# Slot logits in pairs of tiles, and the products with d in one group, in a fused attention and soft-MoE kernel

## What is computed

```python
# attention, 8 batches, 8 heads, 576 tokens, head dim 64; keys and values are pooled by 8 to 72
k_p = k.reshape(B, H, 72, 8, D).mean(axis=3); v_p = ...same...
attn = softmax(q @ k_p.T / sqrt(D))                 # 576 x 72 for each head
x = concat_heads(attn @ v_p)                        # 4608 x 512
# soft MoE, 32 slots
logits = x @ phi                                    # 4608 x 32
d = softmax(logits over the tokens)                 # one column for each slot
slot_in = d.T @ x                                   # 32 x 512
slot_out = relu(slot_in @ w1[e]) @ w2[e]            # 8 experts, 4 slots each
c = softmax(logits over the slots);  x = c @ slot_out
# SoLU layer
h = x @ w_in;  u = h * softmax(h);  out = layernorm(u) * g_ln @ w_out
```

## Time and profile before

| | us |
|---|---|
| median of 3 executions | 486.39 (486.37 to 488.03) |
| the profiled execution | 485.29 |
| its span in the trace | 483.4 |
| PE busy in the span | 442.7 |
| ACT busy | 251.1 |
| DVE busy | 318.9 |
| POOL busy | 271.1 |

### The profile page before, as it was taken

The page is one execution under the profiler, slowest core; times in us unless marked ns, Lnnn a source line. Parts: engine busy times, 40 slices in busy tenths (PEclk is TensorE's granted clock), DMA queues, the critical chain, the costliest instruction groups (busy, mean ns, idle before and its releaser), DMA issues.

```text
span 483.4 us, 10639 instructions
## 1 busy us (share of the span) xinstructions
PE 442.7 (92%) x3845; PEld 357.2 (74%) x3845; DVE 318.9 (66%) x518; ACT 251.1 (52%) x553; POOL 271.1 (56%) x359
## 2 busy tenths in 40 slices
PE   1879999999999997778886999999999999999996
PEld 0867888888888874456655888887878888888885
DVE  7666776868768772735408898767677777777411
ACT  2364758676686752110226765556556665666310
POOL 0397687777888230053812434657576666666540
PEclk9998999999999997898998999999999999999999
DMA  8969897798989447899800016666666666666652
GB/s 264 292 149 293 297 311 213 287 268 299 319 217 322 171 159 259 308 358 397 315 1 0 23 45 133 135 126 134 128 131 135 132 135 135 133 134 132 135 121 48
DMA packets 125296, 91.75 MB, mean 190 GB/s; under 512 B 104776, under 2 KB 104784, under 8 KB 123216
## 3 DMA queue, kind: packets, MB, share of 16 engines
q1 hardware_dynamic: 125264, 91.32, 68.2%
HBM read 66.13 MB, written 9.44 MB: 156 GB/s over the span
## 4 chain that ended last, share of the span: by engine, by line
PE 70%; SPq 11%; DVE 7%; issue 3%; DMA 3%; ACT 3%; POOL 2%; DVEq 0%
SPq L423 10%; PE banks L1373 9%; PE banks L1375 9%; PE banks L1374 9%; PE banks L1065 8%; PE banks L1117 5%; PE banks L1053 4%; PE banks L1133 3%; PE banks L1285 3%; PE banks L1169 3%; PE banks L1350 2%; PE banks L1097 2%; PE banks L1265 2%; PE banks L1141 2%; PE banks L1073 1%
## 5 line engine op out<-in xcount | busy, mean ns | idle before, releaser
L1373 PE MATMUL banks<-wo_hi,uh 128*128 128x512 f32 x288 | 112.5, 391 | 0.0
L1374 PE MATMUL banks<-wo_lo,uh 128*128 128x512 f32 x288 | 112.1, 389 | 0.0
L1375 PE MATMUL banks<-wo_hi,ul 128*128 128x512 f32 x288 | 112.0, 389 | 0.0
L537 POOL TENSOR_TENSOR ul<-u_col,uh 128x1024 fp32r<-128x1024 f32 x30 | 72.1, 2405 | 30.5 <-ACT uh L566 30.4
L457 POOL TENSOR_TENSOR attn<-attn,srec 128x576 f32<-128x576 f32 (+1 forms) x40 | 45.9, 1148 | 59.3 <-DVE srec L802 59.3
L734 ACT ACTIVATE sq<-u,usum 128x1024 f32<-128x1024 f32 x36 | 41.5, 1153 | 41.6 <-DVE u L986 41.5
L1375 PEld LDWEIGHTS banks<-wo_hi,ul 128*128 128x128 f32 x288 | 54.0, 188 | 11.3
L1374 PEld LDWEIGHTS banks<-wo_lo,uh 128*128 128x128 f32 x288 | 54.1, 188 | 11.1
L1373 PEld LDWEIGHTS banks<-wo_hi,uh 128*128 128x128 f32 x288 | 54.1, 188 | 11.1
L976 DVE TENSOR_REDUCE nmax<-banks 128x1 f32<-128x1024 f32 x36 | 43.6, 1220 | 20.0 <-PE banks L1350 20.0
L1065 PE MATMUL banks<-kblk,qT 128*128 128x144 f32 (+1 forms) x320 | 49.9, 302 | 4.8 <-issue 2.4
(11 more groups left out here) (159 smaller groups left out, 753.7 us busy)
## 6 DMA issues: line engine op xcount, KB each, us to landing
wslot<-in_moe_w SPq DMA_DIRECT2D x15, 2048.0 KB, 9.9
u_col<-u_blk SPq DMA_DIRECT2D x240, 64.0 KB, 2.1
qb<-in_q SPq DMA_DIRECT2D x32, 256.0 KB, 6.8
out<-osb SPq DMA_DIRECT2D x32, 256.0 KB, 2.6
kraw<-in_k SPq DMA_DIRECT2D x8, 640.0 KB, 8.9
vraw<-in_v SPq DMA_DIRECT2D x8, 640.0 KB, 5.8
kraw<-in_k SPq DMA_DIRECT2D x8, 512.0 KB, 7.9
vraw<-in_v SPq DMA_DIRECT2D x8, 512.0 KB, 3.9
```

What stands on the lines that cost most here:

```text
L537: pool.tensor_tensor(ul[par][:, :, :].rearrange("p c (q t) -> p (c q) t", q=4), v, uh[par][:, :, :].bitcast(F32).rearrange("p c (q t) -> p ...
L1373: pe.matmul(ps[4 + par], uh[par][:, c, :], wo_hi[:, c, :], start=(c == 0), stop=False)
L1374: pe.matmul(ps[4 + par], uh[par][:, c, :], wo_lo[:, c, :], start=False, stop=False)
L1375: last = pe.matmul(ps[4 + par], ul[par][:, c, :], wo_hi[:, c, :], start=False, stop=(c == FC - 1))
```

## The change

`GROUPS` puts the tiles of a batch into (0,1), (2,3) and (4). The transposed attention `aT` and the copy `lt` become single buffers with room for two tiles. `lt_t`, `lt_evac`, `l_t` and `logit_evac` run once for a group, in steps 2, 4 and 5 instead of all five; for a pair the five matmuls of `lt_t` have 256 columns, `lt_evac` copies 256 columns, and `l_t` is two matmuls. In steps 1 and 3, where `lt_t` stood ahead of `aT_t`, `aT_t` itself now waits for the copy of the tile before. `dat_t` runs for all five tiles at once in step 3, ahead of the scores of that step; its three places of before are gone. `kT_t` moves ahead of `lmax_t` in step 1. Loads that waited for the old counts wait for the new ones. ACT's stream keeps its order and loses `lt_evac` in steps 1 and 3.

```diff
+GROUPS = [(0, 1), (2, 3), (4,)]
-        lt = [bump(f"lt{i}", [P, P]) for i in range(2)]
+        lt = bump("lt", [P, 2 * P])
-        aT = [bump(f"aT{i}", [P, NB, P]) for i in range(2)]
+        aT = bump("aT", [P, NB, 2, P])
...
@@ ACT
-            def lt_evac(tile):
-                n = ROWS[tile[2]]
-                act.wait_ge(sem("lt_ps"), num(tile) + 1)
-                copy(lt[bit(tile)][:, 0:n], b_lt[:, 0:n]).then_inc(sem("lt_sb"), 1)
+            def lt_evac(b, par, g):
+                act.wait_ge(sem("lt_ps"), groups(b, g) + 1)
+                cols = slice(0, 2 * P) if g < 2 else slice(bit((b, par, 4)) * P, bit((b, par, 4)) * P + ROWS[4])
+                copy(lt[:, cols], b_lt[:, cols]).then_inc(sem("lt_sb"), 1)
...
             def step(b, par, t, first, last):
...
-                if not (first and t == 0):
-                    lt_evac(ahead(b, par, t - 1))
+                if t in (2, 4, 5):
+                    lt_evac(b, par, group(t - 1))
...
@@ DVE
-                    sub_max(ahead(b, par, t + 2), None if t != 3 or first else dat_count(b - 1, 0))
+                    sub_max(ahead(b, par, t + 2), None if t != 3 or first else b)
-                if not (first and t == 0):
-                    logit_evac(ahead(b, par, t - 1))
+                if t in (2, 4, 5):
+                    logit_evac(b, group(t - 1))
...
@@ PE
             def aT_t(tile):
...
+                if t in (1, 3):
+                    pe.wait_ge(sem("aT_sb"), g * 2)
                 pe.wait_ge(sem("attn_ready"), g + 1)
...
+            def lt_t(b, par, g, early=False):
+                tiles = [(b, par, t) for t in GROUPS[g]]
+                pe.wait_ge(sem("aT_sb"), num(tiles[-1]) * 2 + 2)
+                if g == 0:
+                    pe.wait_ge(sem("vphi_sb"), b + 1)
+                if not early:
+                    pe.wait_ge(sem("l_sb"), groups(b, g))
                 for k, m in enumerate(BLOCKS):
+                    q = k % 4
+                    if len(tiles) == 2:
+                        o, i = b_lt[32 * q:32 * (q + 1), 0:2 * P], aT[0:m, k, :, :].rearrange("p a n -> p (a n)")
+                    else:
+                        c, n = bit(tiles[0]), ROWS[tiles[0][2]]
+                        o, i = b_lt[32 * q:32 * (q + 1), c * P:c * P + n], aT[0:m, k, c, 0:n]
+                    last = pe.matmul(o, vphi[par][0:m, k, :], i, start=(k < 4), stop=(k + 4 >= NB), tile_position=(0, 32 * q))
                 last.then_inc(sem("lt_ps"), 1)
...
             def step(b, par, t, first, last):
...
                     qT_t(ahead(b, par, t + 3))
-                if t == 4 and not first:
-                    dat_t(b - 1, 1 - par, (4,))
+                if t == 3 and not first:
+                    dat_t(b - 1, 1 - par)
                 if not (last and t + 2 >= TILES):
                     scores(ahead(b, par, t + 2))
+                if t == (2 if first else 1) and not last:
+                    kT_t(b + 1)
                 if not first:
                     if t == 1:
                         lmax_t(b - 1, 1 - par)
                     if t == 2:
                         mb_t(b - 1, 1 - par)
-                    if t == 3:
-                        dat_t(b - 1, 1 - par, (0, 1))
                     if t == 5:
                         slot_t(b - 1, 1 - par)
-                if t == (2 if first else 1) and not last:
-                    kT_t(b + 1)
-                if not (first and t == 0):
-                    lt_t(before, first and t == 1)
+                if t in (2, 4, 5):
+                    lt_t(b, par, group(t - 1), first and t == 2)
                 aT_t(tile)
-                if not (first and t == 0):
-                    l_t(before)
+                if t in (2, 4, 5):
+                    l_t(b, par, group(t - 1))
                 if t == 2 and not first:
                     v72_t(b)
-                if not first:
-                    if t == 3:
-                        dat_t(b - 1, 1 - par, (2, 3))
-                    if t == 4:
-                        datT_t(b - 1)
+                if t == 4 and not first:
+                    datT_t(b - 1)
```

More of the change, by code:

```diff
@@ L281, in c4_batches, with group, groups @@
             return range(2 * (e - 4), 2 * (e - 3)) if e >= 4 else range(0)
-        def dat_count(b, t):
-            return b * 3 + (1 + t // 2)
+        def group(t):
+            return t // 2
+        def groups(b, g):
+            return b * len(GROUPS) + g
         def made(i, k):
@@ L673, in _ @@
             datT_evac(B - 2)
-            lt_evac((B - 1, 1, 4))
+            lt_evac(B - 1, 1, 2)
             d_exp(B - 1)
@@ L1120, in aT_t, with l_t @@
                         last.then_inc(sem("aT_ps"), 1)
[L1122 to L1127, removed]
+            def lt_t(b, par, g, early=False):
+                tiles = [(b, par, t) for t in GROUPS[g]]
+                pe.wait_ge(sem("aT_sb"), num(tiles[-1]) * 2 + 2)
+                if g == 0:
                     pe.wait_ge(sem("vphi_sb"), b + 1)
                 if not early:
-                    pe.wait_ge(sem("l_sb"), g)
+                    pe.wait_ge(sem("l_sb"), groups(b, g))
                 for k, m in enumerate(BLOCKS):
-                    g = k % 4
-                    last = pe.matmul(b_lt[32 * g:32 * (g + 1), 0:n], vphi[par][0:m, k, :], aT[bit(tile)][0:m, k, 0:n],
-                                     start=(k < 4), stop=(k + 4 >= NB), tile_position=(0, 32 * g))
-                last.then_inc(sem("lt_ps"), 1)
[L1137 to L1141, removed]
+                    q = k % 4
[5 more added lines that the diff above has]
+                    last = pe.matmul(o, vphi[par][0:m, k, :], i, start=(k < 4), stop=(k + 4 >= NB), tile_position=(0, 32 * q))
+                last.then_inc(sem("lt_ps"), 1)
+            def l_t(b, par, g):
+                pe.wait_ge(sem("lt_sb"), groups(b, g) + 1)
+                for n, t in enumerate(GROUPS[g]):
+                    c = bit((b, par, t)) * P
+                    last = pe.matmul(b_lt[0:ROWS[t], 2 * P + n * SLOTS:2 * P + (n + 1) * SLOTS], lt[:, c:c + ROWS[t]], fold4[:, :], start=True, stop=True)
+                last.then_inc(sem("l_ps"), 1)
             def lmax_t(b, par):
@@ L1159, in mb_t, with dat_t @@
                 pe.matmul(b_tail[:, 0:SLOTS], slot_max[par][0:SLOTS, :].to_broadcast([SLOTS, P]), ident[0:SLOTS, 0:SLOTS], start=True, stop=True).then_inc(sem("mb_ps"), 1)
-            def dat_t(b, par, tiles):
-                if 0 in tiles:
-                    pe.wait_ge(sem("d_ready"), b + 1)
-                for t in tiles:
+            def dat_t(b, par):
+                pe.wait_ge(sem("d_ready"), b + 1)
+                for t in range(TILES):
                     n = ROWS[t]
@@ L1241, in _ @@
             steps(pe, step)
-            lt_t((B - 1, 1, 4))
+            lt_t(B - 1, 1, 2)
             slot_t(B - 2, 0)
-            l_t((B - 1, 1, 4))
+            l_t(B - 1, 1, 2)
             lmax_t(B - 1, 1)
             mb_t(B - 1, 1)
-            for tiles in ((0, 1), (2, 3), (4,)):
-                dat_t(B - 1, 1, tiles)
+            dat_t(B - 1, 1)
             datT_t(B - 1)
```

29 lines of the change are left out of this document (15 added, 14 removed).

## The result

The changed kernel takes 503.76 us (median of four executions, 501.67 to 507.65), the kernel before beside it 486.44 (486.37 to 488.03): a ratio of 1.036, 95% interval 1.029 to 1.043. The forecast was 496.6 with a range up to 502, so the direction is right and the size is short by 7.2 us. The profiled execution took 504.44 us, with a span of 502.4 against 483.4.

A forecast was written before the change was run, and what follows sets the result against it. PE looked like the bound, but ACT's program order was to delay `l_t` of step 4: six passes at 1.56 us (9.4), plus 0.3 and 0.5 for batches 0 and 7, span 493.6, time 496.6 us; range 490 to 502.

The forecast's parts named there:

- the clock to fall: Rival in the loop: PE's new waits lower its clock, 1.7 us a pass, 507 us (502 in half the passes); chance 0.09.

The follow-up runs named there:

- e2: The kernel before with only the products with d in one group ahead of the scores of step 3; 505.88 us, ratio 1.042.
- e4: The changed kernel with `kT_t` back behind `lmax_t` in step 1; 503.61 us, ratio 1.035.
- e1: The changed kernel with the group of products with d behind the scores of step 3 instead of ahead; 493.81 us, ratio 1.014.
- e5: e1 with DVE's subtraction in step 3 waiting only for the products with d of tile 0, not all five tiles; 485.69 us, ratio 0.998.
- e3: The changed kernel with unused transposes added in step 4: three ahead of the scores, eight ahead of `l_t`; 494.79 us, ratio 1.017.
- e10: The changed kernel with only eight unused transposes added ahead of `l_t` of step 4; 494.19 us, ratio 1.017.
- e6: e5 with ACT's copies of pooled k and v a step earlier and `vT_t` right behind the scores of step 3; 485.01 us, ratio 0.995.
- e7: The changed kernel with the products with d in three groups at their old places, pairs and early `kT_t` kept; 487.64 us, ratio 1.003.
- e8: The changed kernel with `vT_t` between products with d and scores, ACT copying vT in step 3 ahead of the exponentials; 491.52 us, ratio 1.008.
- e9: e6 with `v72_t` ahead of `lt_t` in step 2 and ACT's copy of it a step earlier; 482.73 us, ratio 0.993.

## What to carry to other kernels

An engine that is busy 99.6% of a pass may have the others right at its heels: before moving work on it, ask for each consumer how much room there is between the moved work and the next thing that comes back. When work is gathered into one group, look at both ends of it: what stands behind it, and who waits for its first part but is now released by its last. And where a forecast brings a wait into a loop, look in the trace for that same wait elsewhere and read the clock behind it; then give the fall a term in the sum. And when one whole-program time is to prove a gain in a loop, read the other stages of both traces too: here one of them moved by more than the gain.

## What the runs showed of the hardware

I had not expected the clock to fall with PE busy for about 92% of a pass (20.36 of 22.08 us). All five falls in the loop of the changed kernel began behind the 0.99 us wait of step 4, at `vphi` or, behind it, by the scores; with eight transposes of the unit matrix in its place the clock was 1.00 in all six passes. One trace each gives these counts:

| wait ahead of `l_t` of step 4 | kernel: passes of six with a clock below 1.00 |
|---|---|
| 1.20 to 1.21 us | e2: 4 |
| 0.98 to 0.99 us | after: 5; e4: 5 |
| 0.93 to 0.94 us | e1: 3 |
| 0.28 us | e5: 0 |
| filled | e3: 0; e10: 0 |
| none | before: 0; e6: 1; e7: 1; e8: 2 (0.75 us ahead of the scores); e9: 2 |

In e9 it fell in the same place without such a wait:

```profile
82.88 0.63 PE L1155 MATMUL banks<-fold,lt 128*128 128x32 f32 x4
...
83.57 1.90 PE L1104 MATMUL banks<-phi_pair,vpad 128*128 128x32 f32 x16
85.28 1.09 PE L1060 MATMUL banks<-ident,qb 128*128 128x128 f32 x4
86.17 2.13 PE L1072 MATMUL banks<-kblk,qT 128*128 128x144 f32 x8
```

The transposes of q take 1.09 us for 0.6 here and the scores 2.13 for 1.15, and nothing ahead of them waited. So with the long wait the fall came in 17 passes of 24, and in 6 of the 48 others; the wait makes it likely, and is neither always enough nor its only cause. What else brings it on stays open: no run took that apart, and why one pass of e9 falls and the next doesn't is open as well.
